# Three-stage kernel on one core: softmax of block 0 by itself, its convolution taken from the last tap, opening lists written anew, one root moved in the loop

## The reference

```python
# 1: a convolution over 7 taps, with weights of its own for each token and head
w = np.exp(weight_gen - max over taps); w = w / (sum over taps + 1e-9)
out[b, s, h, :] = sum over k of w[b, s, h, k] * x_pad[b, s + k, h, :]      # x_pad: 6 zero rows, then x
# 2: first layer pair, 192 -> 2048 -> 192, on all 8192 tokens
h = x @ w_in
P = a[0] + a[1]*h + a[2]*h**2 + a[3]*h**3
Q = 1 + abs(b[0])*abs(h) + abs(b[1])*h**2
x = (P / (Q + 1e-6)) @ w_out
# 3: RMS norm, then 192 -> 1536 -> 192 with a gate
xn = x / sqrt(mean(x*x) + 1e-6) * rms_g
out = (silu(xn @ w_gate) * (xn @ w_val)) @ w_out2
```

## Time and profile before

| | |
|---|---|
| median of 3 runs | 1410.36 us (1410.08 to 1413.29) |
| profiled execution, its own time | 1408.61 us |
| span of the profiled execution | 1406.8 us |
| PE busy | 1382.7 us (98%) |
| DVE busy | 1167.5 us (83%) |
| ACT busy | 1080.7 us (77%) |
| POOL busy | 390.9 us (28%) |

### The profile page before, as it was taken

One profiled execution on the slowest core, in us unless ns is written; L12 is line 12 of the kernel. 1 busy time (PEld: TensorE's weight loads), 2 busy tenths in 40 slices (PEclk: granted clock), 3 DMA queues, 4 the chain that ended last, 5 costly groups with the idle time before them and its releaser, 6 DMA issues.

```text
span 1406.8 us, 21014 instructions
## 1 busy us (share of the span) xinstructions
PE 1382.7 (98%) x7328; PEld 1235.7 (88%) x7328; DVE 1167.5 (83%) x1522; ACT 1080.7 (77%) x1455; POOL 390.9 (28%) x281
## 2 busy tenths in 40 slices
PE   7988999999999999999999999999999999999999
PEld 6767999899988989989899898989898898898988
DVE  8999989788888888879788888888878888888622
ACT  5988878887787887778787787888778797787521
POOL 3343153314133240423324033241323324000000
PEclk9999999999999999999999999999999999999999
DMA  8300000100100000000000000000010100000000
GB/s 244 79 0 32 1 32 13 32 13 1 43 0 31 11 31 11 0 31 11 31 11 7 36 0 31 11 31 11 0 37 5 31 12 1 12 1 1 12 12 12
DMA packets 12667, 32.41 MB, mean 23 GB/s; under 512 B 1620, under 2 KB 7506, under 8 KB 12624
## 3 DMA queue, kind: packets, MB, share of 16 engines
q1 hardware_dynamic: 11888, 31.65, 7.1%
q10 hardware_dynamic: 736, 0.20, 0.1%
HBM read 25.55 MB, written 6.29 MB: 23 GB/s over the span
## 4 chain that ended last, share of the span: by engine, by line
PE 91%; DVE 7%; ACT 1%; issue 1%; DMA 0%; SPq 0%; DVEq 0%; ACTq 0%
PE dn L876 39%; PE bank L865 10%; PE bank L866 10%; PE bank L867 10%; PE bank L870 10%; PE bank L871 10%; PE bank L885 2%; DVE num L784 1%; DVE num L781 1%; DVE num L797 1%; DVE den L792 1%; DVE num L803 1%; DVE den L782 1%; DMA x_in<-in_x_dram 0%; ACT num L643 0%
## 5 line engine op out<-in xcount | busy, mean ns | idle before, releaser
L876 PE MATMUL dn<-dn_w,num 128*128 128x192 f32 x2048 | 372.7, 326 | 1.2 <-DVE num L803 1.2
L876 PEld LDWEIGHTS dn<-dn_w,num 128*128 128x128 f32 x2048 | 338.8, 190 | 8.1 <-DVE num L803 2.1
L641 ACT ACTIVATE den<-bank,coef 128x512 f32<-128x512 f32 x256 | 175.8, 687 | 168.2 <-PE bank L871 164.8
L876 PE MATMUL dn<-dn_w,glu 128*128 128x192 f32 x1536 | 279.6, 326 | 0.0
L781 DVE TENSOR_TENSOR num<-num,bank 128x512 f32<-128x512 f32 x256 | 174.9, 683 | 105.7 <-ACT num L643 104.6
L876 PEld LDWEIGHTS dn<-dn_w,glu 128*128 128x128 f32 x1536 | 255.1, 190 | 4.2
L797 DVE SCALAR_TENSOR_TENSOR num<-num,coef,seed 128x1024 f32<-128x1024 f32 x128 | 166.8, 1303 | 50.0 <-ACT seed L664 49.5
L643 ACT ACTIVATE num<-bank,coef 128x512 f32<-128x512 f32 x256 | 200.0, 781 | 0.0
L589 POOL TENSOR_TENSOR conv<-conv,prod 128x768 f32<-128x768 f32 x70 | 128.3, 1833 | 222.2 <-DVE den L792 101.3
L782 DVE SCALAR_TENSOR_TENSOR den<-den,coef,bank 128x512 f32<-128x512 f32 x256 | 190.0, 742 | 0.0
L784 DVE SCALAR_TENSOR_TENSOR num<-num,coef,bank 128x512 f32<-128x512 f32 x256 | 190.0, 742 | 0.0
(11 more groups left out here) (124 smaller groups left out, 2028.8 us busy)
## 6 DMA issues: line engine op xcount, KB each, us to landing
x_in<-in_x_dram SPq DMA_DIRECT2D x14, 960.0 KB
out_dram<-y_out SPq DMA_DIRECT2D x15, 384.0 KB, 2.3
w_blk<-in_weight_gen_dram SPq DMA_DIRECT2D x14, 112.0 KB, 2.0
dn_w<-in_moe_w_out_dram SPq DMA_DIRECT2D x1, 1536.0 KB, 10.6
dn_w<-in_moe_w_out_dram SPq DMA_DIRECT2D x1, 1152.0 KB, 18.0
num<-in_moe_w_in_dram SPq DMA_DIRECT2D x1, 768.0 KB, 6.8
num<-in_moe_w_in_dram SPq DMA_DIRECT2D x2, 384.0 KB, 8.3
x_in<-in_x_dram SPq DMA_DIRECT2D x1, 768.0 KB
```

Source lines behind the costliest of these rows:

```text
L641: act.activation(chunk(den, c % 8), h, ACT.Abs, scale=B_RAW[:, 1:2])
L876: done = pe.matmul(banks[:, j // 2, j % 2 * D:(j % 2 + 1) * D], acts[:, j * P:(j + 1) * P], w, start=first and j % 2 == 0, stop=last, skip ...
```

## The change

1. In front, the softmax covers the logits of block 0 alone. The logits of block 1 come with a transfer of their own. Their maximum is taken by DVE ahead of `x_low 0 0`, POOL subtracts it ahead of `third_low`, and the rest stands in the opening lists as `exp 0 1`, `inverse 0 1` and `norm 0 1`.
2. Block 0's rows come in three parts with a semaphore each: own rows, the nearer three of the rows before, the farther three. The products are taken from the last tap to the first, so that the first product needs own rows alone. SP goes on to the weights when the nearer rows are there, and no longer waits for all.
3. POOL zeroes the rows ahead of a sequence, DVE no longer does.
4. All four opening lists are written in another order.
5. In ACT's loop list `root 3 1` stands behind `linear 10 1`, where it stood ahead of `linear 8 1`.

```diff
-silu 6 3, abs 2 1, linear 7 1, ss 0 2, silu 7 3, abs 3 1, silu 8 3, root 2 1, root 3 1, linear 8 1, linear 9 1,
-linear 10 1, square 2 1, silu 9 3, abs 4 1, silu 10 3, linear 11 1, silu 11 3, square 3 1, xn_high 0 2,
+silu 6 3, abs 2 1, linear 7 1, ss 0 2, silu 7 3, abs 3 1, silu 8 3, root 2 1, linear 8 1, linear 9 1,
+linear 10 1, root 3 1, square 2 1, silu 9 3, abs 4 1, silu 10 3, linear 11 1, silu 11 3, square 3 1, xn_high 0 2,
...
 DVE_OPENING = opening("""
-horner 0 0, horner 1 0, horner 2 0, horner 3 0, horner 4 0, horner 5 0, py 0 0, qy 0 0, qy 1 0, py 1 0,
+inverse 0 1, horner 0 0, horner 1 0, horner 2 0, horner 3 0, horner 4 0, horner 5 0, qy 0 0, py 0 0, horner 6 0,
...
 POOL_OPENING = opening("""
-mul 0 1, mul 1 1, mul 2 1, mul 3 1, mul 4 1, low 0 0 < newton 0 0, mul 5 1 < newton 0 0, mul 6 1 < qy 2 0,
+norm 0 1, mul 0 1, mul 1 1, mul 2 1, mul 3 1, mul 4 1, mul 5 1 < newton 0 0, mul 6 1 < newton 1 0,
...
+        def taps_in(blk):
+
+            early = isinstance(blk, int) and blk < 2
+            return w_first[:, blk * SLOTS * HK:(blk + 1) * SLOTS * HK] if early else w_blk[:, :]
...
         def soft(blk):
-            taps, groups = (w_first, 2 * SLOTS * H) if isinstance(blk, int) and blk == 0 else (w_blk, SLOTS * H)
-            return taps[:, :].rearrange("p (a k) -> p a k", k=K), peaks[:, 0:groups], totals[:, 0:groups]
+            return taps_in(blk).rearrange("p (a k) -> p a k", k=K), peaks[:, :], totals[:, :]
...
-            sp.dma_start(w_first[:, :], w_rows[:, 0:2 * SLOTS * HK]).then_inc(wgen_first, 16)
-            load_first(0)
-            sp.wait_ge(x_in_ready, x_count(0))
+            def load_before(miss, slots, done):
+                lo, hi = slots
                 for q in range(0, P, SEQ_P):
-                    sp.dma_start(x_in[q + 1:q + SEQ_P, 0:miss],
-                                 x_rows[q:q + SEQ_P - 1, PER * D - miss:PER * D]).then_inc(x_in_ready, 16)
+                    sp.dma_start(x_in[q + 1:q + SEQ_P, lo * D:hi * D],
+                                 x_rows[q:q + SEQ_P - 1, (PER - miss + lo) * D:(PER - miss + hi) * D]).then_inc(done, 16)
...
+            load_logits(0)
+            load_own(HALO)
+            load_before(HALO, (HALO // 2, HALO), halo_near)
+            load_before(HALO, (0, HALO // 2), halo_far)
+            load_logits(1)
+            sp.wait_ge(halo_near, 32)
             for n in range(BY_DVE):
                 load_piece(n)
...
             pool.affine_select(out=ident[:, :], in_=ident[:, :], compare_op=ALU.not_equal, fill=1.0,
                                base=0, pattern=[[-1, P]], channel_multiplier=1).then_inc(consts, 1)
+            zeros(pool, 0)
...
             zeros(pool, 1)
 
+            peak_taken_off(1, 0)
             third_low()
...
             dve.memset(coef[:, 14:15], EPS_Q)
-            zeros(dve, 0)
             softmax_peak(0, 0)
...
-            def first_product(k):
-                if k == 0:
+            def first_product(n):
+
+                k = K - 1 - n
+                if n == 0:
                     dve.wait_ge(x_in_ready, x_count(0))
-                elif k == 6:
+                elif n == 1:
+                    dve.wait_ge(halo0, 2)
+                    dve.wait_ge(halo_near, 32)
+                elif n == 4:
+                    dve.wait_ge(halo_far, 32)
+                elif n == 6:
                     dve.wait_ge(sum0, 2)
...
             dve.wait_ge(coefs, 2)
+            softmax_peak(1, 0)
             x_low(0, 0)
```

More of the change, by code:

```diff
@@ L88 @@
[L88 to L106, removed]
+up1 7 0 < up1 5 0, up1 8 0 < up1 2 0, tap 1 1, down1 0 0, tap 2 1, up1 9 0 < up1 6 0, down1 1 0,
+up1 10 0 < up1 7 0, up1 11 0 < up1 3 0, down1 2 0, tap 3 1, tap 4 1, up1 12 0 < up1 9 0, tap 5 1, down1 3 0,
@@ L109 @@
 ACT_OPENING = opening("""
[L110 to L124, removed]
+exp 0 1, linear 0 0, linear 1 0, linear 2 0, linear 3 0, table 0 0, linear 4 0, linear 5 0, abs 0 0, root 0 0,
@@ new lines @@
+square 0 0, abs 1 0, linear 6 0, linear 7 0, abs 2 0, root 1 0, square 1 0, root 2 0, square 2 0, linear 8 0,
+piece 4 0, abs 3 0, linear 9 0, linear 10 0, linear 11 0, piece 5 0, root 3 0, abs 4 0, square 3 0, root 4 0,
+square 4 0, linear 12 0, abs 5 0, root 5 0, linear 13 0, piece 6 0, exp 0 2, square 5 0, linear 14 0,
+x_high 0 1, abs 6 0, x_high 1 1, root 6 0, linear 15 0, square 6 0, linear 0 1, linear 1 1, linear 2 1,
+linear 3 1, abs 7 0, piece 7 0, root 7 0, square 7 0, abs 0 1, abs 1 1, root 0 1, square 0 1, linear 4 1,
@@ new lines @@
+linear 5 1, root 1 1, square 1 1, abs 2 1, root 2 1, ss 0 0, linear 6 1, linear 7 1, linear 8 1, linear 9 1,
+square 2 1, linear 10 1, abs 3 1, linear 11 1, root 3 1, xn_high 0 0, xn_high 1 0, abs 4 1, abs 5 1, square 3 1,
+linear 12 1, root 4 1, root 5 1, linear 13 1, linear 14 1, linear 15 1, square 4 1, x_high 0 2, abs 6 1,
+square 5 1, x_high 1 2, silu 0 0, silu 1 0, abs 7 1, silu 2 0, silu 3 0, root 6 1, linear 0 2, linear 1 2,
+root 7 1, linear 2 2, square 6 1, silu 4 0, abs 0 2, square 7 1, linear 3 2, root 0 2, abs 1 2, silu 5 0,
@@ L125 @@
+exp 0 3, linear 4 2, linear 5 2, root 1 2, square 0 2, linear 6 2, linear 7 2, silu 6 0, square 1 2, abs 2 2,
+ss 0 1, silu 7 0, silu 8 0, linear 8 2, linear 9 2, silu 9 0, linear 10 2, root 2 2, abs 3 2, silu 10 0,
+root 3 2, linear 11 2, silu 11 0, square 2 2, square 3 2, abs 4 2, xn_high 0 1, xn_high 1 1, linear 12 2,
+root 4 2, linear 13 2, abs 5 2, linear 14 2, linear 15 2, y 0 0, x_high 0 3, root 5 2,
 """)
 DVE_OPENING = opening("""
-horner 0 0, horner 1 0, horner 2 0, horner 3 0, horner 4 0, horner 5 0, py 0 0, qy 0 0, qy 1 0, py 1 0,
@@ L129 @@
[L129 to L138, removed]
@@ new lines @@
+horner 1 1, horner 2 1, horner 3 1, qy 6 0, py 6 0, qy 7 0, py 7 0, newton 6 0, qy 0 1, newton 7 0, horner 4 1,
+horner 5 1, py 0 1, qy 1 1, py 1 1, newton 0 1, newton 1 1, horner 6 1, xn 0 0, horner 7 1, horner 8 1,
+horner 9 1, horner 10 1, horner 11 1, xn_low 0 0, py 2 1, qy 2 1, xn_low 1 0, newton 2 1, qy 3 1, py 3 1,
+horner 12 1, newton 3 1, horner 13 1, horner 14 1, horner 15 1, x_low 0 2, x_low 1 2, qy 4 1, glu 0 0, qy 5 1,
+py 4 1, peak 0 3, newton 4 1, glu 1 0, py 5 1, newton 5 1, horner 0 2, horner 1 2, horner 2 2, py 6 1, glu 2 0,
@@ L151 @@
+add 1 3 < py 0 2, rms 0 1, mul 3 3 < newton 1 2, add 2 3 < newton 1 2, mul 4 3, add 3 3, mul 5 3, add 4 3,
+mul 6 3, add 5 3,
 """)
@@ L288, in build @@
         small_in = sem("small_in")
-        wgen_first = sem("wgen_first")
+        wgen_first = [sem(f"wgen_first{n}") for n in range(2)]
         wgen_in = sem("wgen_in")
```

88 lines of the change are left out of this document (53 added, 35 removed).

## The result

The changed kernel took 1411.74 us, the median of 22 runs (1411.00 to 1415.68), against 1409.68 us of the kernel before (22 runs, 1408.52 to 1413.29). The ratio is 1.0015, with a 95% interval of 1.0009 to 1.0022: 2.06 us more. That is within the 0.3% called "same" in the prediction, and inside its range; but the sign is other than forecast, and the interval excludes no change.

A forecast was written before the change was run, and what follows sets the result against it. PE was taken to bound the kernel from 132.35 us on, DVE the 109.56 us before. Terms -2.0 + 0.45 - 0.17 + 0.2 = -1.5 us gave 1408.9 us against 1410.36, range 1406.5 to 1412.5.

The forecast's parts named there:

- the hinge: The end of DVE's `horner 15 1`, which frees the bank for PE's `gate 1 0`; a fixed amount of PE work follows.
- The convolution's start: Front: softmax 0.6 us sooner and 1.4 shorter, wait for x 0.3 less; DVE's convolution operations could end 2.3 us sooner.
- The cap by PE's flips: Front: four flips of 2.01 us each, back to back from 8.87, limit the gain to 2.06 us.
- the -2.0: The front's gain as entered in the sum, in us, after PE's flips limit it.
- I take it that the piece comes 2 us sooner and costs nothing: Front: ACT's third weight piece lands 2 us sooner; if no sooner, only 0.5 of the 2.0 us gain is left.
- DVE's three steps are 378 + 353 ns ..., 0.9 with the gaps: Opening, ahead of the first `horner`: block 1's reduction, small sum and reciprocal on DVE take 0.9 us in all.
- the +0.45 for block 1's softmax: Opening: block 1's exponential on ACT and steps on DVE make the first `horner` 0.4 to 0.5 us later.
- `qy`, `py` and `newton`, at +0.2: Stretch from 22.79 to 132.35 us: DVE steps overlapping POOL's, bounded by -0.53 and +1.6 less 0.53 us, taken as +0.2.
- The stretch: From first `horner` to the hinge, 22.79 to 132.35 us: -0.17 for a wait that goes, +0.2 for POOL overlaps.
- The loop: ACT's moved `root 3 1` gains nothing, PE being full: 0 us.
- The gain of the front is lost on the way: Rival: late piece (+1.5) or POOL overlaps (+1) leave the time of before, 1410.4 us; chance 0.21.
- slower by 0.8 to 4.2: Case: PE waits just behind the hinge, where `value 1 0` wants its `silu`; a 2 us wait gives 1411; chance 0.04.

The follow-up runs named there:

- x1: The changed kernel without the addition of 1e-9 ahead of block 1's reciprocal; 1408.55 us, ratio to before 0.9995.
- x2: The changed kernel with block 1's three DVE softmax steps (`inverse 0 1`) moved behind the second `horner`; 1409.92 us, ratio to before 1.0001.
- x3: The changed kernel with `root 3 1` back in its old place in ACT's loop list; 1411.71 us, ratio to before 1.0015.
- y1: x1 with the four opening lists of before, block 1's softmax steps added at their heads; 1408.69 us, ratio to before 0.9992.
- z2: The changed kernel with POOL's `third_low` made to wait for block 1's reciprocal, the addition kept; 1409.46 us, ratio to before 0.9996.
- x4: The kernel before with an unused DVE addition of a constant behind `horner 0 0`, while `third_low` runs; 1411.19 us, ratio to before 1.0006.
- y2: The kernel before with the new opening lists alone, without their steps of block 1's softmax; 1410.42 us, ratio to before 1.0005.
- y4: The kernel before with an unused DVE `tensor_tensor` addition of two SBUF operands behind `horner 0 0`; 1410.33 us in one run.
- y3: x1 without SP's wait for the nearer rows before issuing the weights; 1408.32 us, ratio to before 0.9996.
- z1: The changed kernel without SP's wait and block 1's addition, with the old opening lists headed by block 1's steps; 1407.65 us, ratio to before 0.9986.

## Why the prediction was right or wrong

**What bounds, and the hinge: right.** PE is full behind `gate 1 0`, which follows `horner 15 1` in all twelve kernels, and the rest is the same to 0.3 us. The time follows from the first `horner` and the stretch behind it, as the prediction said.

**The convolution's start: right.** The softmax started 0.56 us sooner (2.88 for 3.44, forecast 0.6) and was 1.33 us shorter (forecast 1.4). The 0.26 us that the prediction set beside the 0.6 is from a fit for transfers that GpSimd issues; these were issued by SP. The first product came at 5.60 (forecast about 5.5), 2.15 us sooner, with 0.22 us of wait for the nearer rows at the second. The cap by PE's flips was wrong in its detail: the warming ended at 7.6 and not at 8.87, and the fourth flip, at 15.11 for 16.96, waited for DVE's sum. It came 1.85 us sooner, so the -2.0 stood to that point.

**"I take it that the piece comes 2 us sooner and costs nothing": wrong.** The nearer rows landed late enough for SP to issue at 6.70, not 5.4, and ACT's third piece started at 15.75, where 14.7 was the limit set. `x_high` waited until ACT was through with it, at 17.14. The fourth piece, on which the prediction spent no word, held ACT for another 1.39 us. The first `up1` was 1.1 us sooner instead of 2.0. This was no accident of one execution. In the six profiles of the new front with SP's wait (after, x1, x2, x3, y1, z2) the pieces were issued between 6.46 and 7.45 us and ACT took up the third between 13.80 and 18.38, at 16.2 in the median. In the four of the old front (before, x4, y2, y4) they were issued between 7.68 and 8.88, and the third was taken up between 16.08 and 16.45: the earlier issue brought it no sooner. For the fourth ACT waited 1.0 to 2.7 us in five of the six, and in none of the four. Why is open; without SP's wait (y3, z1) the third came at 14.60 and 15.15, but y3's median gave back only 0.2.

**"DVE's three steps are 378 + 353 ns ..., 0.9 with the gaps": the step that failed.** They took 3.7 us, from 21.39 to 25.09. The middle one takes 0.18 us alone (x2, z2) and took 2.86 beside `third_low`. Without these 2.68 us DVE would have been ready for the first `horner` at 25.09 - 2.68 = 22.4. ACT's `linear 0` ended at 21.83 + 0.77 = 22.60, so it would have come at 22.6, 0.2 sooner than before, and 2.5 us are the lock's share of the path. In the prediction's sum the +0.45 for block 1's softmax should have read about +3. That this is the cause is shown from four sides: left out (x1, -3.2 us), moved (x2, -1.8), its neighbour moved (z2, -2.3), and made anew in the kernel before (x4, +1.4, with the 1.29 us in its profile). With the lock away the ratios to before are 0.9995 (x1), 1.0001 (x2) and 0.9996 (z2), each with an interval around 1: the lock accounts for the loss, and the forecast gain of 1.5 us is not there without it either.

The prediction had the mechanism in hand and put it in the wrong place. It let VectorE and GpSimd collide in `qy`, `py` and `newton`, at +0.2, and named only operations with two SBUF inputs. Of that kind the profile after shows one, the `py` of 1.56 us at 119.48, about 0.3 us over its line's mean of 1.28, where before lost 0.53: that term was small, but -0.25 where +0.2 was taken. The small `tensor_scalar` has one input in SBUF and writes to SBUF. The Trainium skill's page "SBUF — State Buffer", section "Who interferes with whom", lists `tensor_scalar` among the VectorE operations that can contend with GpSimd, if their operands meet certain conditions, and says that the later one is then blocked for the whole of the other's instruction. The trace agrees, with 2.86 us against 0.18. The page doesn't name the reciprocal; here it ran free, with 0.35 us beside `third_low`. The collision could be read from the prediction's own times: it had `third_low` start when DVE's piece of 1.76 us ends, and DVE's three steps stand right behind that piece. In the profile the piece ended at 20.96 and ACT's high half, for which `third_low` waited last, at 21.08; `third_low` began at 21.16 and DVE's steps at 21.39.

**The stretch: too low.** Forecast -0.17 for a wait that goes, and +0.2 for overlaps; measured +0.8 in the profile and some +0.7 in the kernels with the new lists. DVE is idle for 1.36 of 110.44 us, where it was for 0.59 of 109.56. Most of the difference has a name: DVE's waits in the stretch sum to 0.97 us, against 0.33 before. Three of them are, from DVE's timeline:

```profile
93.71 1.23 DVE L809 SCALAR_TENSOR_TENSOR den<-den,seed 128x1024 f32<-128x1024 f32 x1 [0.47 <-ACT seed L674]
...
114.70 0.69 DVE L798 TENSOR_TENSOR num<-num,bank 128x512 f32<-128x512 f32 x1 [0.16 <-ACT num L653]
...
116.90 0.69 DVE L798 TENSOR_TENSOR num<-num,bank 128x512 f32<-128x512 f32 x1 [0.19 <-ACT num L653]
```

These are `qy 0 1`, waiting for ACT's square, and `horner 10 1` and `horner 11 1`, waiting for `linear`. All seven profiles with the new lists have the latter two, and besides them either the wait of `qy 0 1` (after, x1) or one of `xn_low 0 0` for `xn_high`, 0.6 to 1.1 us (x2, x3, y2, y3, z2), which the prediction had "about even". Their named waits sum to 0.96 to 1.62 us, those of the five with the old lists to 0.16 to 0.33. So with the new order DVE waits for ACT in places where with the old one it did not. PE's granted clock in the stretch was lower too (0.91 for 0.94), but y4, with the old lists, had 0.92 and 0.16 us of such waits. That the medians don't separate the lists stays open.

**The loop: right.** x3 gave 0.03 us. The profile after has 1.0 us of idle PE in the window from 180 to 1300; x3's has none there, and still the same rest of 1274.8 us.

**The rivals.** "The gain of the front is lost on the way" came nearest. One of its reasons occurred, the piece that lands no sooner, and the other was a collision with POOL. But it named the collisions of `qy`, `py` and `newton`, and priced the case at the time of before, where one collision of 2.7 us elsewhere outweighed the whole gain of the front. The time itself falls into "slower by 0.8 to 4.2", to which 0.04 was given for a wait of PE behind the hinge, and that wait did not occur. That the time lies inside the range is owed to the range's width.

The sum by what was measured in the profiles: -2.15 for the start of the convolution, +1.05 lost to the third piece, +0.9 to the fourth piece and block 1's softmax other than the lock (22.6 - 17.75 = 4.85, where before had 22.79 - 18.85 = 3.94), +2.5 for the lock, +0.8 for the stretch, +0.3 for the rest: +3.4, the difference of the two spans. The medians differ by 2.06, as the profiled execution of before lay 1.1 us below its kernel's median and that of after 0.3 above.
